# Shorter spinning matmuls at the start, own sums moved ahead of them, the last first-step visit one slot later, and one more wait on GpSimd

## The reference

```python
for t in range(S):
    cur = einsum(u * k[t], v[t])               # d x e, per batch and head
    y[t] = einsum(r[t], state + cur)
    state = w[t] * state + einsum(k[t], v[t])
x = y as (tokens, 384)
h = x @ w_in;   x = (h * clip(h + 3, 0, 6) / 6) @ w_out
h = x @ w_in2;  out = (h * sigmoid(h)) @ w_out2
```

## Time and profile before

| what | value |
|---|---|
| median of 3 runs | 920.53 us |
| the profiled execution | 919.04 us |
| its span | 917.3 us |
| TensorE busy | 909.3 us, 99% |
| VectorE, ScalarE, GpSimd busy | 465.9, 319.1, 134.6 us |
| granted TensorE clock, all 40 slices of the page | 0.9 or more of full speed |

### The profile page before, as it was taken

One profiled execution on the slowest core, in us unless ns is written; L12 is line 12 of the kernel. 1 busy time (PEld: TensorE's weight loads), 2 busy tenths in 40 slices (PEclk: granted clock), 3 DMA queues, 4 the chain that ended last, 5 costly groups with the idle time before them and its releaser, 6 DMA issues.

```text
span 917.3 us, 15341 instructions
## 1 busy us (share of the span) xinstructions
PE 909.3 (99%) x5932; PEld 774.9 (84%) x5932; DVE 465.9 (51%) x690; ACT 319.1 (35%) x549; POOL 134.6 (15%) x141
## 2 busy tenths in 40 slices
PE   9999999999999999999999999999999999999998
PEld 5778788888888888888888899999989989999997
DVE  7687856646665674666355533333342333332323
ACT  2545333333333333333354532332232333332322
POOL 4133422404231341333000000000000000000000
PEclk9999999999999999999999999999999999999999
DMA  8352132130113212111212000000000000000001
GB/s 233 104 187 96 58 109 61 49 99 22 56 56 102 59 52 83 39 56 46 104 60 82 31 1 1 35 0 0 34 0 0 34 0 0 34 0 0 35 1 35
DMA packets 13791, 47.08 MB, mean 51 GB/s; under 512 B 1984, under 2 KB 3136, under 8 KB 13760
## 3 DMA queue, kind: packets, MB, share of 16 engines
q1 hardware_dynamic: 13760, 46.66, 16.2%
HBM read 41.93 MB, written 4.72 MB: 51 GB/s over the span
## 4 chain that ended last, share of the span: by engine, by line
PE 95%; DVE 2%; issue 1%; ACT 1%; POOL 1%; DVEq 0%; ACTq 0%; POOLq 0%
PE bank L786 14%; PE bank L787 14%; PE bank L788 14%; PE bank L815 7%; PE bank L817 7%; PE bank L816 7%; PE bank L803 7%; PE bank L805 7%; PE bank L804 7%; PE bank L834 3%; PE bank L899 2%; PE bank L862 2%; PE bank L854 2%; PE bank L843 1%; PE bank L826 1%
## 5 line engine op out<-in xcount | busy, mean ns | idle before, releaser
L425 ACT CAST g_hi<-g 128x512 fp32r<-128x512 f32 x192 | 119.6, 623 | 348.3 <-PE bank L817 204.3
L786 PE MATMUL bank<-x_hi,w_hi 128*128 (+1 forms) x576 | 227.4, 395 | 0.0
L788 PE MATMUL bank<-x_hi,w_lo 128*128 (+1 forms) x576 | 225.1, 391 | 0.0
L787 PE MATMUL bank<-x_lo,w_hi 128*128 (+1 forms) x576 | 225.1, 391 | 0.0
L589 DVE TENSOR_TENSOR g<-g,bank 128x512 f32<-128x512 f32 x96 | 66.0, 687 | 233.9 <-ACT g L419 233.9
L596 DVE TENSOR_TENSOR g_lo<-g,g_hi 128x512 fp32r<-128x512 f32 x192 | 144.9, 755 | 1.0 <-ACT g_hi L425 1.0
L815 PE MATMUL bank<-w_hi,g_hi 128*128 128x384 f32 x384 | 129.0, 336 | 1.7 <-DVE g_lo L596 1.7
L786 PEld LDWEIGHTS bank<-x_hi,w_hi 128*128 128x128 f32 x576 | 108.1, 188 | 25.2 <-DVE g L589 1.8
L817 PE MATMUL bank<-w_hi,g_lo 128*128 128x384 f32 x384 | 128.9, 336 | 0.0
L816 PE MATMUL bank<-w_lo,g_hi 128*128 128x384 f32 x384 | 128.6, 335 | 0.0
L788 PEld LDWEIGHTS bank<-x_hi,w_lo 128*128 128x128 f32 x576 | 108.1, 188 | 22.9
(11 more groups left out here) (96 smaller groups left out, 805.8 us busy)
## 6 DMA issues: line engine op xcount, KB each, us to landing
unit_in<-rkv_tm SPq DMA_DIRECT2D x20, 576.0 KB, 5.9
unit_in<-rk_fm SPq DMA_DIRECT2D x22, 448.0 KB, 4.0
unit_in<-w SPq DMA_DIRECT2D x9, 768.0 KB, 4.2
x<-w SPq DMA_DIRECT2D x7, 768.0 KB, 8.2
unit_in<-w_fm SPq DMA_DIRECT2D x23, 226.2 KB, 4.7
out<-tmp SPq DMA_DIRECT2D x5, 768.0 KB, 3.3
x<-rk_fm SPq DMA_DIRECT2D x2, 448.0 KB, 9.5
out<-tmp SPq DMA_DIRECT2D x4, 192.0 KB, 2.4
```

The costliest lines, as they stand in the source:

```text
L425: nc.scalar.copy(g_hi[:, p, :], g[:, p, :]).then_inc(ghi_done, 1)
L786: nc.tensor.matmul(h_ps[j % 2][:, :], wh, xh, start=k == 0, stop=False)
L787: nc.tensor.matmul(h_ps[j % 2][:, :], wh, xl, start=False, stop=False)
L788: last = nc.tensor.matmul(h_ps[j % 2][:, :], wl, xh, start=False, stop=k == KT - 1)
```

## The change

It does five things. The spinning matmuls have 256 columns instead of 512, and nine stand in the warm-up instead of seven. In the holes between the first units their counts change from 2, 3, 2, 2, 2, 2, 2 to 2, 1, 3, 2, 1, 2 in fewer groups, and the second own sums move from behind the first group to directly behind the first outer product. The visit with b = 3 in step 0 moves from slot 13 to 14, its forward scan from slot 12 to 13. The low part of weight chunk 7 moves from slot 13 to 12. And GpSimd's own products of a unit wait, in all steps, until both masks of the unit before are done.

```diff
@@ -38,7 +38,7 @@
 CHUNKS = 2 * FT // 4
 STAGE1, STAGE2 = 2, 3
 FIRST_STAGE = [0, 1, 2, 0, 1, 0, 1, 0]
-WARM_UP = 7
+WARM_UP = 9
 
 
 def build(nc, rk_fm, w_fm, rkv_tm, u_row, w1, w2, out):
@@ -222,15 +222,15 @@
         SCAN, FORWARD, OWN, TURN, SCORES, MASK, OUTER, KEEP, VALUES, STATE, XHI, XLO = range(12)
 
         WHI_SLOTS = {1: 3, 2: 4, 6: 5, 8: 6, 10: 7}
-        WLO_SLOTS = {2: 3, 5: 4, 8: 5, 11: 6, 13: 7}
+        WLO_SLOTS = {2: 3, 5: 4, 8: 5, 11: 6, 12: 7}
 
 
         VISITS = [4, 7, 10, 13, 15]
         SCANS = [2, 5, 8, 11]
         FORWARDS = [3, 6, 9, 12]
-        VISITS0 = [5, 8, 11, 13, 15]
+        VISITS0 = [5, 8, 11, 14, 15]
         SCANS0 = [3, 6, 9, 12]
-        FORWARDS0 = [4, 7, 10, 12]
+        FORWARDS0 = [4, 7, 10, 13]
 
         def run_pieces(slot, first):
             visits, scans, forwards = (VISITS0, SCANS0, FORWARDS0) if first else (VISITS, SCANS, FORWARDS)
@@ -366,6 +366,7 @@
                 m = b % 2
                 rk, w, tm = units[m]
                 pool.wait_ge(tm_loaded[m], 16 * taken(b, c))
+                pool.wait_ge(masked, 2 * a)
                 nc.gpsimd.tensor_tensor(tm[:, 0, :], tm[:, 0, :], tm[:, 1, :], ALU.mult).then_inc(rk_done, 1)
                 pool.wait_ge(rk_done, a - B + 1)
                 pool.wait_ge(stored, 16)
@@ -896,7 +897,7 @@
 
             def spin_matmuls(into, count):
                 for _ in range(count):
-                    nc.tensor.matmul(into[:, :], fwd_add[:, 1:1 + C], fwd_add[:, 1:1 + C].unsqueeze(1).to_broadcast([KROWS, 4, C]),
+                    nc.tensor.matmul(into[:, 0:2 * C], fwd_add[:, 1:1 + C], fwd_add[:, 1:1 + C].unsqueeze(1).to_broadcast([KROWS, 2, C]),
                                      start=True, stop=True)
 
             def first_own(b):
@@ -939,16 +940,15 @@
             first_turn(0)
             first_raw_scores(0)
             first_outer_product(0)
+            first_own(1)
             spin_matmuls(odd, 2)
-            first_own(1)
-            spin_matmuls(odd, 3)
             first_turn(1)
-            spin_matmuls(odd, 2)
+            spin_matmuls(odd, 1)
             first_raw_scores(1)
             first_outer_product(1)
             first_own(2)
             first_values(0)
-            spin_matmuls(even, 2)
+            spin_matmuls(even, 3)
             first_turn(2)
             first_raw_scores(2)
             first_outer_product(2)
@@ -960,7 +960,7 @@
             first_outer_product(3)
             first_values(2)
             pe.wait_ge(own_done, B)
-            spin_matmuls(first_sums, 2)
+            spin_matmuls(first_sums, 1)
             first_values(3)
             spin_matmuls(first_sums, 2)
             pe.wait_ge(added, 2 * B)
```

## The result

The changed kernel takes 913.60 us, the median of 6 runs (913.27 to 915.99); the kernel before, beside it on the same chip, 920.22 us (6 runs, 919.36 to 921.09). The ratio is 0.9933, interval 0.992 to 0.9946: 6.6 us less. The profiled execution took 913.33 us, its span 911.6, which is 5.7 less than the span before. So the two profiles hold 5.7 us of the 6.6; where the other 0.9 lies is a question for the experiments. (In what follows, lines behind L368 are one higher than before.)

A forecast was written before the change was run, and what follows sets the result against it. Spinning matmuls on TensorE that outlast what they cover were taken to bound the beginning; 4.1 us there plus 1.0 in the first step gave 913.9 for the profiled run, plus 1.5 to the median 915.4, range 913.2 to 918.0.

The forecast's parts named there:

- The likeliest case: Whole kernel: beginning gains 4.1 us and first step 1.0, time from 914.4 to 916.6 us, chance 0.52.
- The warm-up: Opening spins on TensorE: end near 7.4 us instead of 9.91, first own sums start near 7.8.
- the next link: Beginning, behind the warm-up: hides a clock rise up to 2 us later, cost nothing, bound 0.3 us.
- The walk: VectorE and GpSimd followed link by link through the beginning: hidden matmuls start at 35.3 instead of 39.4, 4.1 us gained.
- rival B: Beginning: GpSimd holds on through back-to-back instructions, adding 0.9 us at two or three places; 917.5 us, chance 0.15.
- The first step: Step 0: slot 7 and unit 7's turn gain 0.55 + 0.8, 0.4 given back; 1.0 us net, bounds 0.4 and 1.4.
- Both holes: Step 0, TensorE's waits before slot 7's sums (0.55 us) and before the turn of unit 7 (0.8 us) go.
- the give-back: Step 0, sums of slot 14 wait for g_lo of tile 12: 0.4 us lost, bounds 0 and 0.9.
- The difference to the median: Whole kernel: the median lies 1.5 us above the profiled execution, so 913.9 becomes 915.4 us.
- A: Beginning: VectorE goes first, not held up by GpSimd; hidden matmuls at 33.5, gain 5.9 + 1.0, 913.6 us, chance 0.15.
- D: Beginning: loads hold the start and spins covered nothing, so only the first step gains; 919.5 us, chance 0.06.
- C: Beginning: without long spins TensorE's clock falls to 1.2 GHz, hidden matmuls start at 41 to 43; 923 us, chance 0.08.

The follow-up runs named there:

- the repeat: Nothing changed, each kernel run once more: the changed kernel took 914.26 us (ratio 0.9939), the kernel before 919.71 us (ratio 0.9996).
- the run with late own sums: Against the changed kernel, the second own sums moved back behind the first two spinning matmuls after the warm-up: 914.94 us, ratio 0.9948.

## Why the prediction was right

Forecast 915.4 us, range 913.2 to 918.0; measured 913.60. The likeliest case came, and its steps can be followed one by one.

**The warm-up.** Forecast to end near 7.4, own sums 0 near 7.8; measured 7.51 and 7.47 (TensorE didn't wait for a product that ended at 7.41). That a late rise of the clock would be hidden by the next link is what the repeat showed, for a warm-up 0.95 longer.

**The walk.** Scan 1 was forecast to end at 10.10 and ended at 9.89, the forward scan behind it 12.25 and 12.03, keys 1 13.7 and 13.47, masks 0 16.5 and 16.40, forward 2 19.1 and 18.99, queries 2 22.15 and 22.25, forward 3 26.5 and 26.56, masks 3 31.5 and 31.56, x_lo 3 35.0 and 34.93. Hidden matmuls were forecast from 35.1 to 35.6 and began at 35.03. Gain 4.2, forecast 4.1. One link was wrong: keys 2 were to get in between product 3 and diagonal 2 and end at 20.75; they ended at 21.64, since GpSimd kept the pair through both. That is what rival B says, at one place instead of everywhere. It cost nothing in the sum, and that was luck, for the 0.9 came back at once: the walk had let diagonal 2 run in front of queries 2, and with the diagonal done these took 0.68.

**The first step.** Forecast 0.55 + 0.8 - 0.4 = 1.0; measured 1.3: the lead over the kernel before grows by 0.65 at slot 7 and by 0.7 at the turn of unit 7. Both holes went in full; the give-back was 0.2 instead of 0.4, the term that was mis-sized, within its bounds of 0 and 0.9. Alone these parts gave 1.8 in the medians.

**The difference to the median.** The prediction carried the 1.5 us between the profiled execution and the median over to the changed kernel. That was the step that failed, and it makes two thirds of the distance of 1.8 (1.5 - 0.3 = 1.2): 913.9 was forecast for an execution like the profiled one, and 913.33 came, while the changed kernel's median is only 0.3 over its profile. The 1.5 were no property of the chip that goes with every kernel. Part of them was a median of 3 runs that stood high: with more runs the kernel before took 919.7 to 920.2 us, 0.7 to 1.2 over its profile. The rest, as far as the repeat shows it, was a later clock (0.7 at the second hidden matmul) and the hole at unit 4 (0.8 in the matmuls behind it). The first of these the change takes off the path; the second it keeps, as the repeat of the changed kernel shows. That the changed kernel's profile came so near its median in the result was in part luck: in the repeat the same program took 914.26.

**The rivals.** A (913.6) has the measured time by chance: VectorE did not go first, keys 2 show the opposite. D is refuted by the beginning's 4.9 us alone. C's mechanism did happen: the clock fell between 12 and 16 us. The row that spoke against it, the spins left in the holes, decided the price and not the occurrence: with them the low clock lay beside VectorE's work and cost nothing in the profiled execution, without them 4 to 5 us. It isn't always free: of the changed kernel's eleven runs ten took 913.27 to 914.58 us with a mean granted clock of 0.997 to 1.000, and the one with 0.996 took 915.99; that one was not profiled, so what it lost the time to is not shown. Rival C's price was too high as well: it put some 10 us at the low level at all that the change gains, and the run with late own sums, with some 10 us there, lost 0.7 to 1.3. What the prediction lacked was that a fall can stand in a stretch that another engine bounds.

**Still open.** What exactly makes the clock fall. It fell in six of the eight profiles with the new beginning, first between 12 and 13.5 us in four of them, near 14 and 17.5 in the others. Ahead of each first fall stand holes of 0.3 to 1.6 us among small matmuls; but the two that kept the clock have such holes too (0.25, 0.71 and 1.69 in the run with four diagonals on ScalarE, 0.56 twice, 0.92 and 1.03 in the repeat), and in the changed kernel's own profile the holes of 1.14 and 1.04, ahead of 21.79 and 28.14, were followed by no fall.

## What to carry to other kernels

An engine that is 100% busy with work that nobody reads must be counted by what it covers: take the covers away on paper, and walk the chain of the engines behind it, link by link with their measured durations; that gave the gain of the beginning to 0.1 us, with one wrong link that made itself good. A stretch in which filler work stands on the path turns a late rise of the clock into time. One profile of each kernel doesn't give the gain to better than about 1 us: here the first pair held 5.7, and the medians 6.6 and 5.5. And the filler is needed all the same, in the holes and not beside them.

## What the runs showed of the hardware

By the spacing of the spin passes the clock rose at 5.5 us in the changed kernel's profile and at 8.0 in that with four diagonals on ScalarE, where both began to spin at 1.39; in one program too it moves, as fourteen equal passes of 8.52 and 9.25 us show. The granted clock reads 1.00 in the windows between 5 and 8 us although passes of 256 columns are 0.43 apart there, so that this first half-speed stretch is seen in the spacing alone; the later falls stand in both. In these the clock went to 0.50 and stayed for some 3.4 us in the changed kernel and some 10 in the one with late own sums.

A VectorE instruction with two operands in SBUF that finds GpSimd at work waited for the whole of GpSimd's instruction in these rows (keys 2: 2.73 us instead of 0.68, ended 0.54 behind the diagonal), as the Trainium skill has it (SBUF — State Buffer, "SBUF: two separate sides": the shared pair is an exclusive lock for the whole instruction). Who goes next when both wait is not settled by these rows: VectorE's queries 1, asked for at 13.39, worked between product 2 and the diagonal behind it (it ended at 15.14, the diagonal at 16.09); its keys 2 had to let product and diagonal pass.

Eight ScalarE instructions that scale a 128x128 identity by a value per row follow each other at 0.29 us, 2.45 for the eight; GpSimd makes the same diagonal in one instruction of 1.09 us when nothing is beside it.
